# Attention and two feed-forward blocks on one core: a tile's values weighed five steps behind its scores instead of six

## What is computed

```python
def _attn_ref(q, k, v, centroids):            # 2 batches, 8 heads, 768 tokens, head size 64
    q_assign = argmax(q_n @ c_n)              # nearest of 16 normalised centroids, the same for k
    mask = q_assign[:, :, :, None] == k_assign[:, :, None, :]
    scores = where(mask, scale * q @ k.T, -1e9)
    attn = exp(scores - max(scores))
    attn = attn / (sum(attn) + 1e-09)
    return attn @ v

x = attn_out.transpose(0, 2, 1, 3).reshape(1536, 512)
h = (x @ w1) * (x @ w2) @ w3;  x = h @ w_out              # width 1024
h = x @ w_in;  g = maximum(h, 0) + alpha * minimum(h, 0)
return g @ w_out2                                         # width 2048
```

## Time and profile before

| | us |
|---|---|
| median of 3 runs | 809.65 (808.96 to 810.26) |
| the profiled execution | 811.73 |
| its span in the trace | 809.9 |
| TensorE busy | 768.8 (95%) |
| VectorE, ScalarE, GpSimd busy | 428.4, 336.4, 188.6 |
| TensorE busy in 82 to 340 us | 238.49 of 258 |
| TensorE busy in 340 to 810 us | 460.39 of 470 |

### The profile page before, as it was taken

One profiled execution on the slowest core, in us unless ns is written; L12 is line 12 of the kernel. 1 busy time (PEld: TensorE's weight loads), 2 busy tenths in 40 slices (PEclk: granted clock), 3 DMA queues, 4 the chain that ended last, 5 costly groups with the idle time before them and its releaser, 6 DMA issues.

```text
span 809.9 us, 12352 instructions
## 1 busy us (share of the span) xinstructions
PE 768.8 (95%) x4290; PEld 719.6 (89%) x4290; DVE 428.4 (53%) x704; ACT 336.4 (42%) x679; POOL 188.6 (23%) x210
## 2 busy tenths in 40 slices
PE   5999998898998998699999999999999999999998
PEld 4878998798988987699999999999999999999997
DVE  5224996797887988353212214357444443443442
ACT  5224977787787888342212114343112112112111
POOL 2220476766776774500000000000000000000000
PEclk9999998999999999989999999999999999999999
DMA  8734463544645322320000001333001001001001
GB/s 282 155 115 99 106 138 83 138 112 116 142 113 129 93 60 57 97 79 27 1 1 1 0 0 57 99 104 105 1 1 40 0 1 40 0 0 39 1 1 39
DMA packets 63572, 54.07 MB, mean 67 GB/s; under 512 B 31264, under 2 KB 51760, under 8 KB 63536
## 3 DMA queue, kind: packets, MB, share of 16 engines
q1 hardware_dynamic: 63536, 53.59, 25.2%
HBM read 31.50 MB, written 3.19 MB: 43 GB/s over the span
## 4 chain that ended last, share of the span: by engine, by line
PE 78%; DMA 6%; POOL 5%; SPq 4%; DVE 3%; ACT 2%; issue 2%; ACTq 0%; POOLq 0%; DVEq 0%
PE slot L564 57%; PE acc L564 15%; PE slot L627 5%; DMA xo<-xf 3%; DMA inverses<-rec 2%; POOL xf L511 2%; POOL xf L507 2%; PE acc L577 1%; ACT ph L885 1%; SPq L301 1%; DVE pl L1109 1%; SPq L302 1%; PE slot L678 1%; DVE w L1166 1%; SPq L267 1%
## 5 line engine op out<-in xcount | busy, mean ns | idle before, releaser
L564 PE MATMUL slot<-xh,w 128*128 128x384 f32 (+1 forms) x1024 | 276.6, 337 | 0.0
L564 PEld LDWEIGHTS slot<-xh,w 128*128 128x128 f32 x1024 | 187.0, 188 | 2.4
L564 PE MATMUL slot<-xl,w 128*128 (+1 forms) x512 | 172.3, 337 | 0.0
L1003 ACT CAST gh<-gf 128x384 fp32r<-128x384 f32 x64 | 32.9, 514 | 204.2 <-PE acc L564 178.2
L1109 DVE TENSOR_TENSOR pl<-slot,ph 128x384 fp32r<-128x384 f32 x192 | 97.6, 549 | 21.0 <-ACT ph L885 20.7
L1103 DVE TENSOR_REDUCE nm<-slot 128x1 f32<-128x768 f32 x96 | 91.3, 951 | 25.2 <-PE slot L564 24.3
L627 PE MATMUL slot<-ident,pf 128*128 128x128 f32 x576 | 84.7, 282 | 17.3 <-DVE pl L1109 16.9
L564 PEld LDWEIGHTS slot<-xl,w 128*128 128x128 f32 x512 | 96.1, 188 | 2.2
L627 PEld LDWEIGHTS slot<-ident,pf 128*128 128x128 f32 x576 | 69.3, 144 | 29.0 <-DVE pl L1109 25.3
L885 ACT CAST ph<-slot 128x384 fp32r<-128x384 f32 x192 | 83.6, 485 | 24.6 <-PE slot L627 23.7
L877 ACT ACTIVATE pf<-slot,nm 128x768 f32<-128x768 f32 x96 | 87.8, 915 | 9.5 <-DVE nm L1103 9.4
(11 more groups left out here) (121 smaller groups left out, 1116.6 us busy)
## 6 DMA issues: line engine op xcount, KB each, us to landing
stage<-in_moe_w SPq DMA_DIRECT2D x16, 256.0 KB, 3.2
stage<-in_moe_w_in SPq DMA_DIRECT2D x16, 256.0 KB, 2.8
stage<-in_moe_w_out SPq DMA_DIRECT2D x16, 256.0 KB, 3.0
qk<-in_q SPq DMA_DIRECT2D x16, 192.0 KB, 3.7
qk<-in_k SPq DMA_DIRECT2D x16, 192.0 KB, 4.3
vn<-in_v SPq DMA_DIRECT2D x16, 192.0 KB, 3.4
stage<-in_moe_w SPq DMA_DIRECT2D x6, 512.0 KB, 4.8
q<-k SPq DMA_DIRECT2D x16, 192.0 KB, 2.7
```

Of the source, the lines that this page charges most:

```text
L564: return nc.tensor.matmul(o, a, b, start=start, stop=stop)
L1003: copy(gh[j % 2][:, :], gf[j % 2][:, :]).then_inc(gh_done, 1)
```

## The change

```diff
-LT, LW = 4, 6
+LT, LW, LX = 4, 5, 6
...
 def finished(c):
 
-    j, u = divmod(c - T6 - LW, T6)
+    j, u = divmod(c - T6 - LX, T6)
```

## The result

The changed kernel takes 804.28 us (median of 6 runs, 802.97 to 806.20) against 810.20 (808.96 to 812.13) for the kernel before, measured side by side: a ratio of 0.9923, 95% interval 0.9906 to 0.9941. That is 5.9 us less. The forecast was 798.3, 11.4 less: sign right, time within the range, size about half. It lies in the part of the range (801 to 808) that belonged to rival 1, with a chance of 0.24, and not in the forecast's own (794.5 to 801). The profiled execution took 803.81, 802.0 of it span, 7.9 less span than before.

The account below looks back on a forecast made before the run. TensorE, busy 95%, was taken as stalled in attention by ScalarE's late cast of the odd heads. From 809.65 us, 6.1 + 5.0 - 1.2 + 1.5 = 11.4 gave 798.3; range 794.5 to 807.5, the forecast's own part 794.5 to 801 (chance 0.58).

Parts of the forecast that it names:

- rival 1: The clock falls all the same behind the six stalls; 801 to 808 us, chance 0.24.
- The transfer of the odd head: Transfer issued ahead of the q and k loads; ScalarE's cast waits fall from 15.0 to 8.9 us, gain 6.1.
- The clock: Three falls of the granted clock behind TensorE's stalls in attention go away: gain 5.0 us, possibly 0 or negative.
- the prediction's own pair: Three clock falls in attention priced at 5.0 us, against 7.0 for the full shortfall used at the range's lower end.
- The copy in step 11: Even head's output copy moves from step 0 to step 11, behind the stall: cost 0.2 a period, 1.2 us in all.
- The end of attention: The last half's transfer goes ahead of a weight load: gain 1.5 us, bounds 0.5 and 3.
- Start of attention: One weigh enters where VectorE sets the pace: costs nothing, at most 0.7 us.
- v "over 4 us left": GpSimd splits v in step 8 or 2, needed in 11 or 5, with over 4 us left: cost 0.
- What would show it: Profile signs: xo ahead of the loads, fold without transfer wait, six casts waiting about 1.5 us, clock 1.00 through 120 to 310.
- The rule beside rival 2: Work first on the engine with highest occupancy, TensorE at 95%; by it, the prediction said, the change gives nothing.
- rival 2: No change: TensorE's stalls are filled in one place and open in another; 809.7 us, chance 0.09.

Follow-up runs that it names:

- Run 1: Changed kernel with only SyncE's transfer xo put back in its old step: 814.10 us, ratio 1.0045 to the kernel before.
- run 2: Kernel before with only the loads of q and k one step later, behind the odd head's transfer: 802.32 us, ratio 0.9887.
- run 9: Changed kernel with ScalarE's cast of head 1 at the end of step 10, in the last turn still in step 9: 800.74 us, ratio 0.9871.
- run 5: Kernel before with the last weight load of attention issued behind the transfer of the last half: 809.86 us, one run.
- run 7: Changed kernel with ScalarE's cast of head 1 of each turn at the end of step 10 in place of step 9: 799.28 us, ratio 0.9850.
- run 4: Changed kernel with one more, unused GpSimd operation ahead of the odd head's fold: 812.80 us, one run.
- run 11: The changed kernel itself, measured again: 804.22 us, ratio 0.9913 to the kernel before.
- 8: Changed kernel with output copy and transfer left in their old steps, weigh still five steps behind: 881.37 us, one run.

## Why the prediction was right in sign and half in size

- **The transfer of the odd head (6.1): right.** Fold and cast behave as in the sixth period, in every period. Run 1 takes the gain away, run 2 gives it without the rest. The cast's waits fell by 4.8 and not 6.1, because ScalarE now comes to the cast 0.2 us sooner: 1.70 in place of 1.49. Against GpSimd, which sets the time, the term holds: 3.8 us in five periods, and 2.3 in the first. TensorE's sixth stall turned out not to be like the others: with the same wait of the cast it is 0.3 longer (in run 2 1.56 against 1.25, by the matmuls).
- **The clock (5.0): too much.** The step that failed is "after the change the six stalls should all lie near 1.5 to 1.9 us, where I saw none". Stalls of 1.77 by the weight loads, 1.45 by the matmuls, were followed by a fall once in one profile and twice in another. One stall without a fall, at 1.55, and one at 1.91 had carried the claim. The stall of the fifth period, given as 2.3, is 2.01 by the matmuls, as the others in that list are: a stall with a fall behind it was already close to one without. The mean granted clock tells more than single stalls: 0.985 over 33 runs of the kernel before, 0.990 over 10 of the changed one. One less the clock, times the span, is 12.1 us against 7.7. The 4.4 between them are worth that at most, and about 3.1 by the prediction's own pair (falls priced at 5.0 against a shortfall of 7.0). A straight line through time and clock of the 33 runs gives 0.5 us for each 0.001, or 2.6; all three are estimates. That the shorter stalls are what made the clock better is not shown: run 9, with three of the six taken away, had a mean of 0.987. Rival 1 was the nearer account of this term, with a chance of 0.24.
- **The copy in step 11 (cost 1.2): too little.** I took 0.2 a period. Run 2 against the changed kernel gives 0.4, the sum over five periods gives 0.42: 2.5 in six. I had counted half of the later `ph` as hidden by the score. Nothing of it was: `ph` is 0.35 later, and the score behind it 0.38. The cost came out near the 0.5 that I had named as its bound.
- **The end of attention (1.5): 1.9.** Near, and the place in the queue is between 1.1 (run 5) and all of it (run 1). TensorE's wait for `abl` fell further than I said, to 4.49 in place of 5.8.
- **Start of attention (nothing): right** within what the traces resolve.
- **v "over 4 us left": wrong.** The split of v ends at 125.98 and `weigh` uses it at 127.73: 1.75 us, all of it the stall's. It cost nothing in this change. In run 7, without the stall, the split ends 0.64 after TensorE could have started the weight load, and the copy 0.1 after that.
- **What would show it:** the order in the queue, the fold without a wait and the equal casts came as written. The clock at 1.00 through 120 to 310 did not.

Summed up with the measured sizes: 6.1 + 3.1 - 2.5 + 1.9 = 8.6. Measured are 5.9 (4.8 to 7.6) in the first comparison and 7.9 (812.09 - 804.22) in the last. The terms come from single profiles and the clock differs from run to run by several us, so the rest isn't settled to better than that.

The rule beside rival 2, the Trainium skill, page "Perfetto Trace Analysis", section "Identifying the Most-Contended Engine", names TensorE here. As a measure of the room left on TensorE it takes not the busy share of the matmuls (95%) but their work against the peak and the share of the weight loads, which is 89% before and after. It doesn't say that a change which leaves TensorE's work alone gives nothing; that step was mine, and the runs don't bear it out. Nor were the other engines as close to their limits as rival 2 needs: in 82 to 340 us of the kernel before TensorE is busy 92%, VectorE 82%, ScalarE 78% and GpSimd 66%. TensorE's busy time changed by 0.7 us of 768, the time by 6. At 95% busy, the 5% left were still the place to look.

## What to carry to other kernels

Here a small transfer in an in-order queue was as late as what was issued ahead of it: look at the place of such a transfer before touching the arithmetic, and try to move the large loads, not the work. Run 2 did so in two lines, at a ratio no worse than that of the change. Ask of each stall you shorten what it hides: here it hid v's split. Then read off what chain is late next, and move its consumer; a cast ahead of a more urgent one in an engine's list is worth a step of its own. Don't put a price on the clock from a few stalls; take it from the mean over many runs.

## What the runs showed of the hardware

The fall of the granted clock couldn't be told from the idle time ahead of it. By the idle time of the weight loads, TensorE kept 2.4 GHz behind stalls of 2.92 (before, second period) and 2.66 us (run 4, fourth), and fell behind some of 1.77 (changed kernel, run 11). One and the same program, the kernel before, had a mean clock between 0.978 and 0.994 in 33 runs and times between 804.5 and 815.0 us. That spread is larger than most of the effects studied here, and single runs (4, 5, 8) were read for their stalls, not for their times.

The transfer `xo` needed 4.6 us from issue to landing where 384 KB were issued ahead of it. The change didn't make `xo` land faster as a rule: over its 32 transfers the median from issue to landing is 2.2 us before and 2.9 in the changed kernel, the longest 4.6 and 4.1. What it gained is the time of the issue. At the end of attention, with a weight load ahead, copy to fold took 5.6 to 6.3 us (before, runs 1 and 2); with that load behind it, 3.2 to 5.2 (all other runs whose order is so).
